# An attention and feed-forward kernel: reciprocals widened on VectorE and turned in whole transposes, and another order of the opening

## What is computed

```python
q_rot, k_rot = rotate(q), rotate(k)
scores = (1 / sqrt(64)) * q_rot @ k_rot.T
attn = exp(scores - max(scores)); attn = attn / (sum(attn) + 1e-9)
x = attn @ v                       # heads side by side: 2304 x 512
h = x @ w_in                       # 512 x 2048
g = maximum(h, 0) + alpha * minimum(h, 0)
out = g @ w_out                    # 2048 x 512
```

## Time and profile before

| | |
|---|---|
| median of 3 runs | 667.3 us |
| profiled execution, own time | 667.3 us |
| its span | 665.5 us |
| TensorE busy | 654.6 us, 98% |
| VectorE, ScalarE, GpSimd busy | 338.2, 320.3, 266.8 us |
| attention | until about 265 us |
| mean granted clock of TensorE | 0.995 |

### The profile page before, as it was taken

One profiled execution on the slowest core, in us unless ns is written; L12 is line 12 of the kernel. 1 busy time (PEld: TensorE's weight loads), 2 busy tenths in 40 slices (PEclk: granted clock), 3 DMA queues, 4 the chain that ended last, 5 costly groups with the idle time before them and its releaser, 6 DMA issues.

```text
span 665.5 us, 14995 instructions
## 1 busy us (share of the span) xinstructions
PE 654.6 (98%) x5570; PEld 561.9 (84%) x5570; DVE 338.2 (51%) x779; ACT 320.3 (48%) x730; POOL 266.8 (40%) x254
## 2 busy tenths in 40 slices
PE   7899999999999999999999999999999999999998
PEld 6787778778877777988899999999999999999996
DVE  4577887778887773456423332333233323332222
ACT  2688888888888884333332223222322232223223
POOL 3756788888776214222222222222222222222222
PEclk9799999999999999999999999999999999999999
DMA  6596455445545426000010001000100010001001
GB/s 150 147 230 175 112 127 134 116 105 121 119 107 118 97 91 253 1 0 1 1 49 0 1 0 48 1 1 0 47 0 0 0 47 0 0 0 48 1 0 48
DMA packets 73309, 41.58 MB, mean 62 GB/s; under 512 B 59812, under 2 KB 64292, under 8 KB 72740
## 3 DMA queue, kind: packets, MB, share of 16 engines
q1 hardware_dynamic: 72978, 40.62, 23.3%
q10 hardware_dynamic: 274, 0.16, 0.1%
HBM read 22.95 MB, written 4.72 MB: 42 GB/s over the span
## 4 chain that ended last, share of the span: by engine, by line
PE 96%; DVE 1%; ACT 1%; DMA 0%; SPq 0%; issue 0%; POOL 0%; DVEq 0%
PE banks L756 30%; PE banks L785 30%; PE banks L700 9%; PE banks L598 9%; PE banks L674 5%; PE banks L625 3%; PE banks L696 3%; PE banks L572 2%; PE banks L647 2%; PE banks L652 1%; PE banks L553 1%; DMA cos_sb<-in_cos 0%; PE banks L580 0%; PE banks L655 0%; PE banks L643 0%
## 5 line engine op out<-in xcount | busy, mean ns | idle before, releaser
L520 POOL TENSOR_TENSOR g_lo<-g,g_hi 128x384 fp32r<-128x384 f32 (+1 forms) x98 | 99.7, 1017 | 304.8 <-ACT g_hi L941 301.5
L1105 DVE TENSOR_SCALAR g<-banks,alpha_sb 128x384 f32<-128x384 f32 (+1 forms) x98 | 59.7, 609 | 249.2 <-ACT pos L932 249.2
L756 PE MATMUL banks<-x_hi,w_in_lo 128*128 128x384 f32 x384 | 129.3, 337 | 0.0
L756 PE MATMUL banks<-x_hi,w_in_hi 128*128 128x384 f32 x384 | 129.3, 337 | 0.0
L756 PE MATMUL banks<-x_lo,w_in_hi 128*128 128x384 f32 x384 | 129.0, 336 | 0.0
L932 ACT ACTIVATE pos<-banks 128x384 f32<-128x384 f32 x96 | 47.2, 491 | 169.2 <-PE banks L756 169.2
L785 PE MATMUL banks<-w_out_hi,g_hi 128*128 128x512 f32 x288 | 114.9, 399 | 0.3
L785 PE MATMUL banks<-w_out_hi,g_lo 128*128 128x512 f32 x288 | 112.9, 392 | 0.0
L785 PE MATMUL banks<-w_out_lo,g_hi 128*128 128x512 f32 x288 | 111.9, 389 | 0.0
L941 ACT ACTIVATE g_hi<-g 128x384 fp32r<-128x384 f32 (+1 forms) x98 | 50.9, 519 | 116.5 <-DVE g L1108 116.5
L828 ACT ACTIVATE prob<-prob,nmax 128x576 f32<-128x576 f32 x128 | 98.3, 773 | 1.3 <-DVE prob L996 1.1
(11 more groups left out here) (80 smaller groups left out, 918.2 us busy)
## 6 DMA issues: line engine op xcount, KB each, us to landing
q_swap<-q_nat SPq DMA_DIRECT2D x32, 256.0 KB, 3.8
k_swap<-k_nat SPq DMA_DIRECT2D x32, 144.0 KB, 3.2
out<-stage SPq DMA_DIRECT2D x18, 256.0 KB, 2.0
raw_q<-in_q SPq DMA_DIRECT2D x32, 128.0 KB, 2.9
raw_k<-in_k SPq DMA_DIRECT2D x32, 128.0 KB, 2.6
raw_v<-in_v SPq DMA_DIRECT2D x32, 128.0 KB, 2.3
w_in_raw<-in_moe_w_in SPq DMA_DIRECT2D x4, 1024.0 KB, 6.9
w_out_raw<-in_moe_w_out SPq DMA_DIRECT2D x8, 512.0 KB, 6.9
```

What stands on the lines that cost most here:

```text
L520: nc.gpsimd.tensor_tensor(g_lo[f % 2][:, part], g[f % 2][:, part], g_hi[f % 2][:, part].bitcast(F32), ALU.subtract).then_inc(g_lo_done, 1)
L756: mm = nc.tensor.matmul(h_ps[f % 2], w[:, j, cols], xx[:, j, :], start=(step == 0), stop=(step == 3 * CT - 1))
L1105: nc.vector.tensor_scalar(g[f % 2][:, part], h_ps[f % 2][:, part], 0.0, alpha_sb[:, f:f + 1], ALU.min, ALU.mult).then_inc(neg_done, 1)
```

## The change

Three things.

1. The reciprocals are computed in two parts. first_sums takes the tiles REM and A0 to A3 in the pair's own period (add and reciprocal after the maxima of B1, the copy after the flat copy of PA2), last_sums takes B0 to B3 in the next (add and reciprocal where reciprocals stood, the copy after the maxima of A3). In each, VectorE copies four columns of inv, each repeated 64 times, into one half of a new tile inv_wide [128, 4, 128]. U_INV is then four transposes of 128x128 in place of the eight products.
2. In period 0 U_Q is turned after A2, its high part is taken after the exponentials of A1 and its low part after the maxima of A2. B2 is computed before PA0. U_Q and U_K of this period go to banks 6 and 7, U_MIXED to bank 5 (OPENING_BANK); U_K waits for U_Q's evacuation, and PA2 for U_K's.
3. In period 0 the product of zeros stands before A1 to B1 only, and goes to bank 4.

```diff
+OPENING_BANK = {U_Q: 2, U_K: 3, U_MIXED: 1}
...
-        if u == U_QREM or (u == U_Q and not (isinstance(p, int) and p < 0)):
+        if u == U_QREM or (u == U_Q and not (isinstance(p, int) and p <= 0)):
...
-                if is_opening(p) and n > 1:
-                    run_in(1)
+                if is_opening(p) and A_TILES[0] < n <= B_TILES[1]:
+                    run_in(1, 4)
...
+                    if is_opening(p):
+                        pe.wait_ge(evac[bank_of(p, U_Q)], evac_count(p, U_Q))
                     turned_in(p, 1)
...
-                if u != U_KQREM and has_prev(p):
-                    pe.wait_ge(inv_done, p)
+                if u == U_INV:
+                    pe.wait_ge(wide_done, p * 2)
+                elif u == U_MIXED and has_prev(p):
+                    pe.wait_ge(inv_done, p * 2 - 1)
...
                     for i in range(QT):
-                        for r, n in zip(HEADS, (A_TILES[i], B_TILES[i])):
-                            mm = nc.tensor.matmul(bank[r, i * P:(i + 1) * P], inv[:, par, n:n + 1].to_broadcast([P, D]),
-                                                  ident[:, :], start=True, stop=True)
+                        mm = nc.tensor.transpose(bank[:, i * P:(i + 1) * P], inv_wide[:, i, :], ident[:, :])
...
                 score(p, t, A_TILES[2])
+                if is_opening(p):
+                    turn(p, t, U_Q)
                 score(p, t, A_TILES[3])
...
                 if is_opening(p):
-                    turn(p, t, U_Q)
                     turn(p, t, U_K)
                     spread(p, t, U_MIXED)
+                    score(p, t, B_TILES[2])
                 spread(p, t, U_INV)
                 turn_two(p, t, U_PA[0])
-                score(p, t, B_TILES[2])
+                if not is_opening(p):
+                    score(p, t, B_TILES[2])
                 score(p, t, B_TILES[3])
...
+            def first_sums(p, t, step):
+
+                if not has_now(p):
+                    return
+                par, n = t % 2, p * 2 + 1
+                tiles = slice(REM_TILE, B_TILES[0])
+                if step == 0:
+                    dve.wait_ge(exp_done, p * TILES + B_TILES[0])
+                    nc.vector.tensor_tensor(rsum[:, par, tiles], rsum[:, par, tiles],
+                                            tiny[:, :].to_broadcast([P, B_TILES[0]]), ALU.add).then_inc(sum_done, 1)
+                elif step == 1:
+                    dve.wait_ge(sum_done, n)
+                    nc.vector.reciprocal(inv[:, par, tiles], rsum[:, par, tiles]).then_inc(inv_done, 1)
+                else:
+                    dve.wait_ge(inv_done, n)
+                    if has_prev(p):
+                        dve.wait_ge(turned, unit_count(p, U_INV))
+                    nc.vector.tensor_copy(inv_wide[:, :, LOW], inv[:, par, A_TILES[0]:B_TILES[0]].unsqueeze(2)
+                                          .to_broadcast([P, QT, D])).then_inc(wide_done, 1)
...
+                    dve.wait_ge(inv_done, n)
+                    nc.vector.tensor_copy(inv_wide[:, :, HIGH], inv[:, par, tiles].unsqueeze(2)
+                                          .to_broadcast([P, QT, D])).then_inc(wide_done, 1)
...
                 maxima(p, t, A_TILES[2])
+                if is_opening(p):
+                    lo(p, U_Q, t)
...
                 maxima(p, t, A_TILES[3])
+                last_sums(p, t, 2)
                 if not is_opening(p):
                     lo(p, U_MIXED, t)
                 maxima(p, t, B_TILES[0])
                 maxima(p, t, B_TILES[1])
                 if is_opening(p):
-                    for u in OF_NEW:
-                        lo(p, u, t)
+                    lo(p, U_K, t)
+                    lo(p, U_MIXED, t)
+                first_sums(p, t, 0)
+                first_sums(p, t, 1)
                 normalise(p, *before, 0)
                 maxima(p, t, B_TILES[2])
                 maxima(p, t, B_TILES[3])
                 flat(p, U_PA[2], t)
+                first_sums(p, t, 2)
                 normalise(p, *before, 1)
```

More of the change, by code:

```diff
@@ L90, in exists_now, with bank_of @@
         return exists(PAIRS if not isinstance(p, int) else p, u)
+    def bank_of(p, u):
+        return OPENING_BANK.get(u, BANK_OF[u]) if isinstance(p, int) and p == 0 else BANK_OF[u]
     def tally(p, u, counted):
@@ L105, in evac_count @@
     def evac_count(p, u):
-        return tally(p, u, [w for w in range(UNITS) if BANK_OF[w] == BANK_OF[u]])
+        if isinstance(p, int):
+            return sum(exists(r, w) for r in range(-1, p + 1) for w in range(UNITS)
+                       if bank_of(r, w) == bank_of(p, u) and (r < p or w <= u))
+        return p * BANK_OF.count(BANK_OF[u]) + (evac_count(PAIRS, u) - PAIRS * BANK_OF.count(BANK_OF[u]))
     def pt_slot(par, head, j):
@@ L186, in build @@
             raw_v = [sb(att, f"raw_v{i}", [P, ST, P]) for i in range(2)]
-            sb(att, "behind_values", [P, CT * CHUNK - 2 * ST * P])
+            inv_wide = sb(att, "inv_wide", [P, QT, P])
+            assert 2 * ST + QT >= CT * MT
             until_prob = used[0]
@@ L236, in by_rows @@
             else:
-                two = banks[:, 6:8, :] if u in (U_QREM, U_KREM) else banks[:, 4:6, :]
+                opens = isinstance(p, int) and p == 0
+                two = banks[:, 6:8, :] if opens or u in (U_QREM, U_KREM) else banks[:, 4:6, :]
                 first = (QT * D) * (u in (U_KREM, U_K))
@@ L360, in swap @@
                 if side == 0:
-                    sp.wait_ge(evac[BANK_OF[U_Q]], evac_count(p - 1, U_Q))
+                    sp.wait_ge(evac[bank_of(p - 1, U_Q)], evac_count(p - 1, U_Q))
                     dst, cols, arrived = q_swap[par], (slice(0, QT * P), slice(0, QT * P)), q_swap_in
@@ L364, in swap @@
                 else:
-                    sp.wait_ge(evac[BANK_OF[U_K]], evac_count(p - 1, U_K))
-                    sp.wait_ge(evac[BANK_OF[U_MIXED]], evac_count(p - 1, U_MIXED))
+                    sp.wait_ge(evac[bank_of(p - 1, U_K)], evac_count(p - 1, U_K))
+                    sp.wait_ge(evac[bank_of(p - 1, U_MIXED)], evac_count(p - 1, U_MIXED))
                     dst, cols, arrived = k_swap[par], (slice(0, HALF), slice(REM + HALF, REM + S)), k_swap_in
@@ L539, in fill @@
                 if not (isinstance(n, int) and n == 0):
-                    pe.wait_ge(evac[BANK_OF[u]], n)
-                return t_ps[BANK_OF[u]]
+                    pe.wait_ge(evac[bank_of(p, u)], n)
+                return t_ps[bank_of(p, u)]
             def turned_in(p, side):
@@ L548, in turned_in, with run_in @@
                     pe.wait_ge(rope_step, (p + 1) * 8 + side * 4 + 4)
-            def run_in(count):
+            def run_in(count, bank=7):
                 for _ in range(count):
-                    nc.tensor.matmul(banks[:, 7, 0:P], blank[:, :], blank[:, :], start=True, stop=True)
+                    nc.tensor.matmul(banks[:, bank, 0:P], blank[:, :], blank[:, :], start=True, stop=True)
             def score(p, t, n):
@@ L563, in score @@
                     for u in OF_NEW:
-                        pe.wait_ge(evac[BANK_OF[u]], evac_count(p - 1, u))
+                        pe.wait_ge(evac[bank_of(p - 1, u)], evac_count(p - 1, u))
                 if not (isinstance(s, int) and s < 2):
@@ L663, in turn_two @@
                 halves = (fill(p, u), fill(p, u + 1))
+                if u == U_PA[2] and is_opening(p):
+                    pe.wait_ge(evac[bank_of(p, U_K)], evac_count(p, U_K))
                 if u in U_PA:
@@ L835, in hi @@
                 act.wait_ge(turned, unit_count(p, last_of(p, u)))
-                bank = t_ps[BANK_OF[u]]
+                bank = t_ps[bank_of(p, u)]
                 nx = (t + 1) % 2
@@ L871, in flat @@
                     ins = nc.scalar.activation(dst, src, ACT.Copy)
-                ins.then_inc(evac[BANK_OF[u]], 1)
+                ins.then_inc(evac[bank_of(p, u)], 1)
             def high_w_out(f):
@@ L902, in period @@
                 exps(p, t, A_TILES[1])
+                if is_opening(p):
+                    hi(p, U_Q, t)
                 exps(p, t, A_TILES[2])
@@ L905, in period @@
                 if is_opening(p):
-                    for u in OF_NEW:
-                        hi(p, u, t)
+                    hi(p, U_K, t)
+                    hi(p, U_MIXED, t)
                 flat(p, U_INV, t)
@@ L1046, in flat @@
                     ins = nc.vector.tensor_copy(dst, src)
-                ins.then_inc(evac[BANK_OF[u]], 1)
-            def reciprocals(p, t, step):
+                ins.then_inc(evac[bank_of(p, u)], 1)
+            def first_sums(p, t, step):
[16 more added lines that the diff above has]
+                                          .to_broadcast([P, QT, D])).then_inc(wide_done, 1)
@@ L1051, in reciprocals, with last_sums @@
+            def last_sums(p, t, step):
                 if not has_prev(p):
                     return
-                par = (t - 1) % 2
+                par, n = (t - 1) % 2, p * 2
```

(21 more changed lines are left out.)

9 lines of the change are left out of this document (5 added, 4 removed).

## The result

| | before | after |
|---|---|---|
| median of 7 runs | 667.51 us | 672.08 us |
| lowest, highest | 667.19, 669.35 | 669.61, 672.84 |
| profiled execution: own time, span | 667.3, 665.5 | 671.37, 669.6 |

The changed kernel is slower: ratio 1.0065, 95% interval 1.0052 to 1.0079. The prediction was 667.8 us with a range to 671.5, so the time lies outside it. Run once more on another chip the ratio was 1.0064 (1.0042 to 1.0086). One execution of the kernel before, on the chip of the first four experiments, took 799 us at a granted clock of 0.75; it is in no ratio.

The account below looks back on a forecast made before the run. TensorE, busy for 98% of the span, was taken to bound the kernel. Twelve blocked periods +4.9 us, four others -2.2 and the opening -2.2 gave +0.5: 667.8 us, range 657 to 671.5.

Parts of the forecast that it names:

- The bound and the block: TensorE bounds; in periods 2 to 13 VectorE's second copy waits for GpSimd's rope add, making U_INV 0.97 us late.
- Rivals 1, 3 and 4: Copy not blocked: 656.1 us, chance 0.22; transposes at 0.070: 666.2, chance 0.10; transposes cost like products: 676.7, chance 0.06.
- Saved: 0.94 - 0.38 = 0.56 us a unit: U_INV on TensorE: eight products of 0.94 us become four transposes of 0.38; saving 0.46 to 0.66.
- Opening: -2.2: Period 0 reordered: U_KREM of period 1 at about 29.6 instead of 32.02; gain 2.2 us, bounds 0 and 2.4.
- I expect no fall of the clock: In the opening TensorE's gap shrinks from 2.2 to 1.5 us, so its clock stays at 1.00.
- rival 2: The clock falls in period 1 and takes the opening's gain: 670.0 us, chance 0.20.
- The sum: Whole kernel: +2.7 us from the periods and -2.2 from the opening make +0.5, so 667.8 us.
- the forecast's own formula: Twelve blocked periods cost 0.97 us less the unit's saving, four others gain that saving, and the opening's gain is subtracted.
- The forecast's own range: Range of the main forecast for the kernel's time, 666.2 to 669.4 us; chance of that forecast 0.42.
- the wide range: Range of 8 in 10 for the kernel, 657 to 671.5 us, reaching to rival 2 with a dear transpose.

Follow-up runs that it names:

- the first four experiments: The reciprocals' part alone 671.95 us, the opening's part alone 666.10; the changed kernel with second copy earlier 663.59, with that copy as a one-path multiplication 663.45.
- The opening alone: The kernel before with only the new opening, keeping its eight products and reciprocals: 666.10 us against 667.73, ratio 0.9978.
- the best version: The changed kernel with the second copy moved behind the copy of U_PB[3] and both small adds in one-input form: 660.00 us, again 660.39.
- the unit alone: The changed kernel with the opening of the kernel before put back, the reciprocals' part kept: 671.95 us against 667.73, ratio 1.0056.
- products of zeros: The changed kernel with early copy and one-input small adds, plus products of zeros in TensorE's three opening rests: 660.45 us, ratio 0.9892.

## Why the prediction was wrong, step by step

**The bound and the block: right.** The copy meets the rope add in the periods named, 2 to 13; it takes 1.50 to 1.57 us there (1.5 forecast), TensorE waits 0.95 to 0.97 (0.97 forecast), and the chain through U_MIXED's bank is the one described. Three experiments show it from three sides: another place, another form, another GpSimd instruction. Here the trace agrees with the rule of the Trainium skill, "SBUF — State Buffer", Who interferes with whom: the copy in the two-port mode waited out GpSimd's instruction, the form that writes out its accumulator (0.42 us) did not. Rivals 1, 3 and 4 are out. One reading of the rows was off: in period 1 the 0.29 us that are left at the copy's place belong to the product with the sines (L453), not to the rope add; the copy took 0.289 us there in the first profiled execution and 1.42 in the second.

**"Saved: 0.94 - 0.38 = 0.56 us a unit": mis-sized, the first failure.** By the prediction's own recipe the whole transposes come every (0.66 - 0.27)/3 = 0.13 us, where I took 0.095 as a middle; four make 0.52. The unit went from 1.03 to 0.59 us, 0.44 saved, below the lower bound of 0.46. The plain 128x128 product (0.120 a record) was the right row, the half transposes (0.070) the wrong one. Over 16 units this is 1.9 us. The Trainium skill, "TensorE: Matmul & The Clock Gate", Terms, would have had 0.06; the trace doesn't bear that out here: one whole fp32 transpose takes 0.13 us, against 0.24 for a plain product, a factor of 1.9 and not four.

**"Opening: -2.2": mis-sized, the second.** Until the start of period 2 the kernel gained 1.33 us, and 0.44 of that is the unit's: 0.9 in place of 2.2. Two steps of it failed. "I expect no fall of the clock": it fell at 25.7 for 6.8 us, as at 25.1 before, in spite of a shorter rest (1.2 us in place of 2.2). This is rival 2 in part, which I had put at 0.20. And a wait was left out: U_KQREM of period 1 goes to bank 5, which PA1 holds until ScalarE has done two exponentials and the copy; I let period 1's first tile start at once after PA2. It started at 28.16, ran at 1.2 GHz and pushed U_KREM to 30.39, where the exponentials alone (the last ended at 29.61) allowed about 29.7. The opening alone tells the two apart: with the same wait, but the clock up until 28.3, U_KREM followed the last exponential by 0.14 us. So the wait cost something only together with the low clock. More was lost behind U_KREM, which was 1.63 us ahead: the clock stayed low until 32.5 (31.9 before), and the turns of U_PB's second pair, at 32.92 against 33.66, were 0.74 ahead.

**The sum.** Forecast and measured, by span: blocked periods +4.9 and +6.55 (0.41 and 0.55 each; with 0.44 saved the forecast's own formula gives 0.53); the three unblocked periods 14 to 16 -1.7 and -1.1; opening and period 1 -2.8 and -1.3. Together +0.5 and +4.1. No term had the wrong sign, but both gains were put too high, the unit's by 1.9 us over its 16 periods and the opening's by 1.3. With these two put right (0.44 and 0.9) the forecast's own formula gives 12 x 0.53 - 4 x 0.44 - 0.9 = +3.7, close to the +4.1 measured. The forecast's own range (666.2 to 669.4) took only the unit's price as uncertain, and the wide range added rival 2 to the dear end of that price, 0.46 us saved; the measured 0.44 lies beyond it. The profiled execution (671.37) is just inside 671.5 and the median 0.6 us outside, which is less than the executions of one kernel differ by.

What stays open: why the opening alone gained 1.5 us on the kernel before and nothing measurable on the best version. The differences in time that go with the mean clock are larger than that between executions of one kernel.

## What to carry to other kernels

Before work is put on VectorE beside a busy GpSimd, look up what GpSimd is in the middle of at that moment, and which unit waits behind the new operation: here 0.28 us of copying became 1.50, and 0.55 us a period was lost in place of 0.44 gained. A small copy or add can be made in a form that doesn't wait (one input, with an accumulator written out; 0.42 us instead of 0.28), or put where GpSimd waits itself. After each wait that is removed the next one shows: the add that had been covered at 14.72 us a period cost 0.48 at 14.29.

## What the runs showed of the hardware that was not expected

- A whole fp32 transpose of 128x128 comes every 0.13 us at 2.4 GHz; half ones (64x128) come in pairs, a pair every 0.070; a plain fp32 product of 128x128x128 comes every 0.24, in two records.
- The low stretch of TensorE's clock in the opening isn't in the same place in every execution of one kernel. The best version was profiled twice: it lay at 27.5 to 34.3 in one execution, at 9.1 to 12.5 and again at 29.6 to 33.0 in the other. The changed kernel had it at 25.7 to 32.5 both times. In the other kernels it lay at 11.3 to 14.7 and again at 25.0 to 35.2 (the unit alone), at 28.3 to 31.7 (the opening alone), and at 10.8 to 14.2 (products of zeros). The time goes with the mean clock: the kernel before took 665.4 to 665.8 us at a mean clock of 1.000, 667.0 to 668.1 at 0.995, and 669.8 to 670.1 at 0.990; the changed kernel 669.6 to 669.7 at 1.000. At an equal mean clock of 1.000 the change costs 4 us, at 0.995 about the same.
